# An expert layer's second product, with tokens or with features on the partitions: a mixture-of-experts kernel on Trainium2

## The reference, cut to what matters

```python
logits = x @ w_gate
expert_idx = np.argmax(logits, axis=1)
# disp[e] holds the tokens of expert e, in their order, up to capacity
h = np.maximum(np.einsum('ecd,edf->ecf', disp, w1), 0.0)
y = np.einsum('ecf,efd->ecd', h, w2)
out[i] = gate_w[i] * y[expert_idx[i], pos[i]]   # for each kept token i
```

## Time and profile before

| | us |
|---|---|
| median of 3 runs | 689.39 (684.84, 689.39, 689.58) |
| the profiled execution | 684.15 |
| its span, from the first to the last instruction | 682.4 |
| PE busy in the span | 617.6 |
| DVE busy | 526.7 |
| ACT busy | 439.3 |
| start of the first expert's first product | 488.83 |

### The profile page before, as it was taken

The page is one execution under the profiler, slowest core; times in us unless marked ns, Lnnn a source line. Parts: engine busy times, 40 slices in busy tenths (PEclk is TensorE's granted clock), DMA queues, the critical chain, the costliest instruction groups (busy, mean ns, idle before and its releaser), DMA issues.

```text
span 682.4 us, 13478 instructions
## 1 busy us (share of the span) xinstructions
PE 617.6 (91%) x4302; PEld 552.5 (81%) x4302; DVE 526.7 (77%) x1017; ACT 439.3 (64%) x728; POOL 288.6 (42%) x294
## 2 busy tenths in 40 slices
PE   5778797999999999999999999998889889889895
PEld 3555796897997888988979879796789779878895
DVE  5999998989989979979899880146196865866862
ACT  2567477779678596796796877547186357356440
POOL 0377367467376575574765766505001001101111
PEclk9988599899999999999999999999899999899999
DMA  5965500000000000000000000233788474474300
GB/s 174 373 284 215 213 6 5 25 5 5 24 9 1 27 7 18 11 5 23 4 4 16 0 13 5 96 136 124 255 323 289 150 264 160 161 267 156 136 12 21
DMA packets 17792, 68.62 MB, mean 101 GB/s; under 512 B 1998, under 2 KB 6606, under 8 KB 15056
## 3 DMA queue, kind: packets, MB, share of 16 engines
q1 hardware_dynamic: 16000, 63.27, 25.3%
q0 software_dynamic: 1744, 4.73, 2.0%
HBM read 54.33 MB, written 14.45 MB: 101 GB/s over the span
## 4 chain that ended last, share of the span: by engine, by line
PE 52%; ACT 14%; issue 10%; POOL 10%; DMA 6%; DVE 6%; POOLq 1%; ACTq 0%; DVEq 0%; SPq 0%
PE p_a L1280 7%; PE p_o L1242 6%; PE p_b L1280 5%; PE p_s L1204 5%; PE p_b L1302 4%; POOL arena L677 3%; PE p_t L1221 3%; PE p_b L1304 3%; PE p_b L1303 3%; DVE w_lo L565 3%; DMA out_rows<-h_sb,own_number 3%; DMA out_rows<-turns,own_number 2%; ACT arena L842 2%; PE p_t L1474 2%; POOL w_out_lo L716 2%
## 5 line engine op out<-in xcount | busy, mean ns | idle before, releaser
L374 DVE MAX8 top<-arena 128x8 f32<-128x576 f32 x288 | 201.0, 744 | 7.4 <-ACT arena L842 7.4
L377 DVE MATCH_REPLACE8 arena<-top,arena 128x576 f32<-128x576 f32 x216 | 158.5, 740 | 0.0
L677 POOL TENSOR_TENSOR arena<-arena,pen 128x576 f32<-128x576 f32 x72 | 100.6, 1419 | 58.1 <-ACT pen L849 58.1
L1242 PE MATMUL p_o<-arena,probsT 128*128 128x65 f32 (+1 forms) x720 | 91.0, 273 | 6.2 <-ACT probsT L869 4.5
L1242 PEld LDWEIGHTS p_o<-arena,probsT 128*128 128x128 f32 (+1 forms) x720 | 85.8, 191 | 13.4 <-ACT probsT L869 7.5
L869 ACT COPY probsT<-p_t 128x384 f32<-128x384 f32 x108 | 51.2, 480 | 52.8 <-PE p_t L1221 52.7
L1302 PE MATMUL p_b<-w_out_lo,g_hi 128*128 128x512 f32 x144 | 62.9, 437 | 5.3 <-DVE g_lo L404 3.5
L1280 PE MATMUL p_a<-xT,wff 128*128 128x128 f32 x512 | 65.9, 283 | 0.0
L1221 PE MATMUL p_t<-ident,arena 128*128 128x128 f32 x324 | 55.9, 284 | 11.0 <-ACT arena L861 11.0
L1280 PE MATMUL p_b<-xT,wff 128*128 128x128 f32 x512 | 64.3, 279 | 0.0
L1280 PEld LDWEIGHTS p_a<-xT,wff 128*128 128x128 f32 x512 | 60.7, 195 | 2.8 <-issue 2.4
(11 more groups left out here) (187 smaller groups left out, 1348.3 us busy)
## 6 DMA issues: line engine op xcount, KB each, us to landing
arena<-in_w SPq DMA_DIRECT2D x8, 2048.0 KB, 9.0
wff<-in_w SPq DMA_DIRECT2D x8, 2048.0 KB, 8.4
slot_rows<-y_now SPq DMA_DIRECT2D x1, 4626.0 KB, 14.5
wff<-in_w_out SPq DMA_DIRECT2D x1, 4096.0 KB, 12.1
wff<-in_w_in SPq DMA_DIRECT2D x1, 4096.0 KB, 21.9
wff<-slot_rows SPq DMA_DIRECT2D x8, 385.5 KB, 8.8
arena<-in_vones SPq DMA_DIRECT2D x2, 1300.0 KB, 16.5
q_sb<-in_q SPq DMA_DIRECT2D x36, 64.0 KB, 1.9
```

What stands on the lines that cost most here:

```text
L374: nc.vector.max(best, src).then_inc(top_step, 1)
L377: nc.vector.match_replace(work[:, a, :], best, src, LOWEST).then_inc(top_step, 1)
L677: nc.gpsimd.tensor_tensor(s_sb[:, t, :], s_sb[:, t, :], pen[:, t % 2, :], ALU.subtract).then_inc(masked, 1)
L1242: last = mm(p_o[q, lo:lo + n], probsT[:, g % 2, P * c + q.start:P * c + q.stop], vones[b][:, p, at:at + n], start=(k == 0), stop=(k == PAI ...
```

## The change

The second product is made the other way round. The inner activations (now in two tensors, he_hi and he_lo) are stationary, 96 tokens at a time, and w2 moves over 512 columns. Of the three combinations each is one matmul: 48 per expert where there were 64. The result has tokens on the partitions and accumulates in the bank p_oe[s] that `scale_rows` read before, so units 4 and 5, their cross copies and sums and `turn_back` are gone. `keep` and its buffers are gone too: the scaling and the scatter read weight and number from the rows' buffer. So the load of rows now waits for the scatter of the expert two earlier, and SP issues w1, rows, w2 in this order. The high parts of w1 and w2 have one home each: `high_w1` of the next expert waits for all of this expert's first product, and `high_w2` for all of the previous expert's second product. `unit_ready` is named `he_ready` and `sum_made` `he_sum_made`, with four counts per expert.

```diff
-        w1_hi = [over("w1_hi0", arena, 0, W1), over("w1_hi1", w_out_hi, 0, W1)]
-        w2_hi = [over("w2_hi0", arena, 4096, W2), over("w2_hi1", w_out_hi, 4096, W2)]
+        w1_hi = over("w1_hi", arena, 0, W1)
+        w2_hi = over("w2_hi", arena, 4096, W2)
...
@@ SyncE, expert_loads @@
-                wait(sp, kept, E - 1)
+                wait(sp, he_ready, 4 * E - 4)
+                sp.dma_start(w1_raw[j], w1_d[e]).then_inc(w1_in[j], 16)
+
+                wait(sp, out_sent[j], 16 * NSB * turn)
                 expert_rows(e, j, r)
 
-                wait(sp, unit_ready, UNITS * E - 2 * UNITS + UP_UNITS)
-                sp.dma_start(w1_raw[j], w1_d[e]).then_inc(w1_in[j], 16)
-
-                wait(sp, unit_ready, UNITS * E - UNITS)
+                wait(sp, oe_ready, NSB * E - NSB)
                 sp.dma_start(w2_raw[j], w2_d[e]).then_inc(w2_in[j], 16)
...
@@ VectorE, the new expert @@
+                low_w2(E, j, 0)
+                low_w2(E, j, 1)
+                sum_he(E, 0, n)
+                for c in range(1, 4):
+                    sum_he(E, c, n)
+                    low_he(E, c - 1, n)
+                low_w2(E, j, 2)
+                low_he(E, 3, n)
+                low_w2(E, j, 3)
+                if more:
+                    low_x(E + 1, n)
+                    low_w1(E + 1, 1 - j)
+
                 wait(dve, out_sent[j], 16 * NSB * turn)
                 for s in range(NSB):
                     wait(dve, oe_ready, NSB * E + s + 1)
-                    nc.vector.tensor_scalar(oe[j][0:n, s, :], p_oe[s][0:n, :], own_weight[0:n, j, s:s + 1],
+                    nc.vector.tensor_scalar(oe[j][0:n, s, :], p_oe[s][0:n, :], rows[j][0:n, s, DM:DM + 1],
                                             None, ALU.mult).then_inc(oe_copied, 1)
-            def keep(E, j, turn, n):
-                wait(dve, rows_in[j], 16 * (turn + 1))
-                wait(dve, out_sent[j], 16 * NSB * turn)
-                nc.vector.tensor_copy(own_weight[0:n, j, :], rows[j][0:n, :, DM])
-                nc.vector.tensor_copy(own_number[0:n, j, :], rows[j][0:n, :, DM + 1].bitcast(I32)).then_inc(kept, 1)
...
@@ ScalarE @@
+            def high_w1(E, j, turn):
                 wait(act, w1_in[j], 16 * (turn + 1))
+                wait(act, he_ready, 4 * E)
...
+                    wait(act, oe_ready, NSB * E)
+                nc.scalar.copy(w2_hi[:, 2 * c:2 * c + 2, :], w2_raw[j][:, 2 * c:2 * c + 2, :]).then_inc(w2_hi_made, 1)
...
             def expert(E, j, turn, n, more=True):
+                high_w2(E, j, turn, 0)
+                high_w2(E, j, turn, 1)
                 copy_cross(E, 0, n)
+                high_w2(E, j, turn, 2)
+                for c in range(1, 4):
+                    copy_cross(E, c, n)
+                    high_he(E, c - 1, n)
+                    if c == 1:
+                        high_w2(E, j, turn, 3)
                 high_he(E, 3, n)
                 if more:
                     high_x(E + 1, n)
+                    high_w1(E + 1, 1 - j, turn + j)
...
@@ TensorE, behind the first product and turn_rows @@
+                wait(pe, oe_copied, NSB * E)
+                for c in range(4):
+                    wait(pe, he_lo_made, 4 * E + c + 1)
+                    wait(pe, w2_lo_made, 4 * E + c + 1)
+                    for s in range(NSB):
+                        for f in (2 * c, 2 * c + 1):
+                            cols = slice(m * f + n * s, m * f + n * s + n)
+                            a, b = (he_hi[:, cols], he_lo[:, cols]), (w2_hi[:, f, :], w2_lo[j][:, f, :])
+                            mm(p_oe[s][0:n, :], a[0], b[1], start=(f == 0), stop=False)
+                            mm(p_oe[s][0:n, :], a[0], b[0], start=False, stop=False)
+                            last = mm(p_oe[s][0:n, :], a[1], b[0], start=False, stop=(f == FC2 - 1))
+                        if c == 3:
+                            last.then_inc(oe_ready, 1)
```

More of the change, by code:

```diff
@@ L521, in gated, with low_w1 @@
                 nc.vector.tensor_tensor(h_sb[:, part], h_sb[:, part], turns[:, part], ALU.mult).then_inc(g_ready, 1)
-            def low_w1(E, j, pieces=range(4)):
-                for c in pieces:
+            def low_w1(E, j):
+                for c in range(4):
                     wait(dve, w1_hi_made, 4 * E + c + 1)
@@ L590, in low_he, with expert @@
+                nc.vector.scalar_tensor_tensor(he_lo[:, part], he_sum[c % 2][:, 0:4 * n], 0.0,
+                                               he_hi[:, part].bitcast(F32), ALU.max,
                                                ALU.subtract).then_inc(he_lo_made, 1)
-            def scale_rows(E, j, turn, n):
+            def expert(E, j, turn, n, more=True):
+                low_w2(E, j, 0)
[10 more added lines that the diff above has]
+                    low_w1(E + 1, 1 - j)
@@ L650, in _ @@
                 low_x(NE, ROUNDS[1][1])
-                keep(NE, 0, NE // 2, ROUNDS[1][1])
                 expert_round(dve, 1, expert)
@@ L1096, in _ @@
             high_g(last, 3)
-            def high_w1(E, j, turn, pieces=range(4)):
+            def high_w1(E, j, turn):
                 wait(act, w1_in[j], 16 * (turn + 1))
-                for c in pieces:
+                wait(act, he_ready, 4 * E)
+                for c in range(4):
                     part = slice(256 * c, 256 * c + 256)
-                    nc.scalar.copy(w1_hi[j][:, :, part], w1_raw[j][:, :, part]).then_inc(w1_hi_made, 1)
+                    nc.scalar.copy(w1_hi[:, :, part], w1_raw[j][:, :, part]).then_inc(w1_hi_made, 1)
             high_w1(0, 0, 0)
@@ L1140, in high_he @@
                                      ACT.Relu).then_inc(he_hi_made, 1)
             def expert(E, j, turn, n, more=True):
-                begin = isinstance(E, int) and E % NE == 0
-                after = (E + 1, 1 - j, turn + j)
-                if not begin:
-                    copy_cross(E - 1, 5, n)
+                high_w2(E, j, turn, 0)
+                high_w2(E, j, turn, 1)
                 copy_cross(E, 0, n)
-                if more and not begin:
-                    high_w1(*after, (0,))
@@ L1164, in expert @@
+                for c in range(1, 4):
[3 more added lines that the diff above has]
+                        high_w2(E, j, turn, 3)
                 high_he(E, 3, n)
-                if begin:
-                    high_w2(E, j, turn, 3)
                 if more:
                     high_x(E + 1, n)
-                    high_w1(*after, range(4) if begin else (2, 3))
-                    high_w2(*after, 0)
-                copy_cross(E, 4, n)
@@ L1172, in expert @@
-                if more:
-                    for c in range(1, 4):
-                        high_w2(*after, c)
-                if not more:
-                    copy_cross(E, 5, n)
+                    high_w1(E + 1, 1 - j, turn + j)
             high_x(0, ROUNDS[0][1])
@@ L1477, in expert @@
                                 mm(bank_f[:, 0:m], w1_lo[j][:, k, cols], high_x, start=False, stop=False)
[L1478 to L1481 removed]
+                                last = mm(bank_f[:, 0:2 * m], w1_hi[:, k, cols], both_x, start=False, stop=True)
@@ L1503, in expert @@
-                turn_back(E, 0, n)
-                if not more:
-                    turn_back(E, 1, n)
+                wait(pe, oe_copied, NSB * E)
+                for c in range(4):
+                    wait(pe, he_lo_made, 4 * E + c + 1)
[9 more added lines that the diff above has]
+                            last.then_inc(oe_ready, 1)
```

153 lines of the change are left out of this document (25 added, 128 removed).

## The result

| | before | after |
|---|---|---|
| median of 4 runs each, us | 687.12 (684.84 to 689.58) | 667.42 (665.96 to 668.93) |
| the profiled execution, us | 684.15 | 668.93 |
| its span, us | 682.4 | 667.2 |

The ratio after to before is 0.971, with the interval 0.966 to 0.977: faster by 2.9%. The forecast was 668.

The account below looks back on a forecast made before the run. PE, nearly the bound, lost some 3 us per expert to DVE's scatter wait. From 488.83, first expert 20.76 + 2.0, six rounds 127.3 and last 20.15 gave 659.0; span 664.3, execution 666.0, plus 2 made 668; range 659 to 684.

Parts of the forecast that it names:

- What bounded the kernel: Expert rounds of 24.3 us: PE nearly the bound, some 3 us lost per expert to DVE's `keep` awaiting a slow scatter.
- PE gains 1.1 us of work per expert: Second product on PE: 48 matmuls over 512 columns, 10.99 us, replace 32 pairs, 9.17, and eight transposes, some 0.7.
- The new circle: Between experts: scatter lands, rows load, PE turns them; PE stalls 0.4 to 0.5 us per expert, 2.7 us in all.
- T: The end of the second product of expert E, from which the prediction times scatter, rows and w2 parts.
- The 0.45 us of stall per round: PE's wait for turned rows in six rounds, which makes each 20.76 + 0.45 us.
- the thinnest cover: w2's preparation on ACT and DVE: first sum ready 0.4 us before PE's unit 2; cost 0, bounds 0 to 1 us per expert.
- Stall 2.0 us: First expert's first product: PE waits at unit 2 for a sum behind w2's casts and subtractions; 0 if the load is earlier.
- The 2 us put on top: Added to 666.0 us, giving 668, because the median before lay 5.2 us above the profiled execution, for unknown reasons.
- The first: Rival: scatter meets a load and takes 9.09 us, rows come 6.2 us later each round, 703 us; chance 0.09.
- The second: Rival: loads end only at about the second product's end, 2 to 3 us lost per round, 678 to 684; chance 0.09.
- the third: Rival: w2 parts late through register work ahead of the loop's waits, 1 us per expert, 673 us; chance 0.09.
- The fourth: Rival: PE was the bound, 0.255 us matmuls and today's stalls, 676 us plus stalls; chance 0.03.

Follow-up runs that it names:

- e1_keep_later: Kernel before, with `keep` moved in DVE's order from the end of the expert before to right behind the scaling: 665.36 us, ratio 0.967.
- e5_w1_behind_scatter: Kernel before, `keep` in its old place, SP issuing each next w1 load only when the scatter in between has landed: 665.39 us, one run.
- e6_two_homes: Changed kernel with w1_hi and w2_hi in two homes again and the two waits for the single home taken out: 674.11 us, one run.
- e2_first_w2_later: Changed kernel with the first expert's w2 casts and low parts put one behind each sum, as in the kernel before: 664.55 us, ratio 0.967.
- e10_changed_again: Changed kernel with no edit, five rounds beside two other kernels on one chip: 666.12 us, ratio 0.970.
- e3_rows_last: Changed kernel with SP issuing w1, w2, rows instead of w1, rows, w2: 702.32 us, one run.
- e4_wait_back: Changed kernel with DVE again waiting, ahead of the next w1's low parts, for the scatter that `keep` waited for: 669.74 us, one run.
- e7_mixed: Kernel before with `keep` moved to right behind the scaling, and the new second product for the last expert alone: 664.58 us, ratio 0.965.
- e11_keep_later_again: Kernel before with `keep` moved to right behind the scaling, run again without edit beside two other kernels on one chip: 665.07 us, ratio 0.970.

## Why the prediction was right

**What bounded the kernel.** Right for five of the six rounds, and shown from two sides: e1_keep_later takes the waiter out of the scatter's way, e5_w1_behind_scatter takes the load out of it, and each brings these five from 24.5 to 20.4 us. The first round was read wrongly as one of the same kind. Its 23.44 us came from the first expert's w2, not from `keep`, and both experiments leave it at 23.3 to 23.5.

**PE's work.** The matmuls over 512 columns run at 0.231 us from start to start (10.87 us for 47 distances from 546.33 to 557.20), against the 0.229 taken and the 0.213 and 0.255 of the bounds. The round without stalls is 20.95 us, against 20.76. The term "PE gains 1.1 us of work per expert" was twice too large. The clean rounds of the old orientation take 20.4 us, so the work grows by 0.5 to 0.6. The step that failed took the old second product from 32 pairs and eight transposes alone, 9.9 us; the rest of the old round was never measured free of stalls, because no such round stood in the trace of before. It did not touch the forecast, which was made from the new round.

**The new circle.** Right in its order and nearly in its times. With T at 536.6 us: scatter issued at T + 1.7 (1.8 forecast), rows issued at T + 5.0 (4.7), turned at T + 9.1 without a wait, where T + 9.4 was forecast and T + 9.0 wanted. The 0.45 us of stall per round did not come, since PE's own round is 0.2 us longer and the rows took 3.8 us in the median and not 4.25. Together that is 21.08 against 21.21 us. The estimate of 2.5 us for the scatter and 2.9 for the rows did not come: they took 3.54 and 3.8.

**DVE and ACT, the thinnest cover.** The first sum ends at T + 4.0, against 3.9 forecast and 4.4 wanted; PE never waits for it in a round. That POOL's second scatter would be drawn out to 1.5 us by DVE's subtractions was not in the working. It cost nothing here, and 7 us in e6_two_homes.

**First expert.** The stall was forecast at 2.0 us and measured at 2.2, by the chain named. What was missed is the clock behind it, another 2 us, although showed that very thing behind another stall. The term "Stall 2.0 us" measured 4.0 here. The slow clock is not certain behind such a wait: in e6_two_homes PE waits 2.1 us at the same place, the clock stays at 1.00 and the first product takes 11.6 us. e2_first_w2_later gives back 3.9 us of span.

**The sum.** Predicted gain of the rounds 18.5, measured 19.3; cost of the first expert 1.9, measured 4.0; the start taken as unchanged, measured 1.1 later (it varies from execution to execution: 488.95 in e10_changed_again, the same program); the last stretch 1.5, measured 1.0. The span is 667.2 us against 664.3, the profiled execution 668.93 against 666.0. The 2 us put on top for the spread made up for it, by luck and not by reasoning: the after runs spread by 3 us and their median is 1.5 below the profiled one.

**The rivals.** The first is true as a mechanism (e3_rows_last, 702.32) and did not apply, as the loads were in by the time of the scatter. The second and the third did not occur. The fourth, that PE was the bound and nothing is saved, is half true in another way: PE is the bound now, and the new orientation saves it no work in a round.

## What to carry to other kernels

When a rewrite removes a wait, look for the smallest edit of the old kernel that removes the same wait, before the gain is credited to the rewrite: here one moved call, or one wait on a load, was worth the whole change. Price a stall on PE as a range, with and without slow clock behind it, from rows of the same trace, and check what is in flight on the DMA engines when a small, late transfer starts. A wait that looks like pure cost can keep two engines apart, so after taking one away read the durations of the neighbours' instructions as well as the waits.

## What the runs showed of the hardware that was not expected

- POOL's issue of the same 96-row scatter took 0.92 us alone, 1.40 to 1.57 us when a subtraction of DVE from two SBUF inputs had started just before it, and 3.56 us when a run of two such began 0.42 us after it. (Of the other scatters of e6_two_homes one took 2.17 and two some 1.04.) In the long case it ended 0.8 us behind the end of DVE's run. In the changed kernel a scatter started half a microsecond into an equal run of two was held for 0.6 us only, and the runs do not tell why that one got through between the two.
- A scatter of 96 rows took 3.54 us to land where the weight loads were in, 7.20 us beside a w2 load and 9.09 beside a w1 load. The last two are the second expert's; in the changed kernel that one was issued at 538.32, and SP, which waits for it, issued the rows 3.3 us later.
- PE's granted clock was 0.50 behind single waits of 2.2 us in the first expert (1.7 in e10_changed_again and e4_wait_back) and of 3.3 to 4.5 us in e3_rows_last. It stayed at 1.00 in the first stretch of e1_keep_later, which holds waits of 1.5 and 0.8 us, and behind a wait of 2.1 us in the first expert of e6_two_homes. It fell to 0.50 behind the same waits of 1.5 and 0.8 us in e7_mixed. The runs do not tell what decides between the two.
- From the last scatter's issue to the end of the span went 3.3 us in the earlier trace rows, 3.7 in the changed kernel (663.48 to 667.2) and 5.3 in e1_keep_later, but 3.3 in e11_keep_later_again, the same program as e1_keep_later. The start of the experts moved as well, 490.69 in the one and 488.79 in the other. The causes were not looked for. Together they are 3.9 us between two executions of one program, more than the differences between the leaders.
